# A mixture-of-experts kernel in which the second layer's first tile takes in the last routing of the first layer, and in which two and three tiles may start before all rows are there

## The chip, the cores and the metric

The kernel runs on one core of a Trainium2 chip. A core has five engines with an instruction stream each: PE (TensorE, matrix products; PEld is its weight load), DVE (VectorE), ACT (ScalarE), POOL (GpSimd) and SP (SyncE, which here only issues DMAs). Engines meet by semaphores. The metric is the device time of one execution in microseconds (us), lower is better.

## The reference

Three stages follow each other on 14336 tokens (4 batches of 3584) of 192 features. First a causal convolution of 7 taps, with softmax weights, one set of taps for each of 8 groups of features:

```python
w = exp(weight - max); w = w / (sum(w) + 1e-9)
x[b, s, head h] = sum_k w[h, k] * x_pad[b, s + k, head h]
```

Then a first layer of 8 experts, which only tokens with a positive skip score go through (the others pass unchanged), and a second layer of 8 experts for all tokens:

```python
# layer one, only where x @ w_skip > 0
e = argmax(x @ w_gate);  p = softmax(x @ w_gate)[e]
x = x + p * (relu(x @ w1[e]) @ w2[e])
# layer two, all tokens
e = argmax(x @ w_gate2); p = softmax(x @ w_gate2)[e]
out = p * sigmoid(x @ w_output_gate)[e] * (relu(x @ w1b[e]) @ w2b[e])
```

w1 is 192 x 1024 and w2 is 1024 x 192 for each expert, all float32. Each expert's tokens must be known before its products can be made in tiles, so both layers sort tokens by expert.

## The kernel before, in words

The program has three parts.

**The front** takes the tokens in 16 groups (4 batches of 4) of 7 x 128 tokens. For a group PE does the convolution (`conv`), ACT copies it to the buffer `rows` (`rows_out`, L521), PE transposes it and multiplies by the routers, ACT copies the scores (L557), PE turns them back (`scores_of`), DVE finds the expert, the gate and, with counts from PE (`ranks_of`), the row in a bucket that each token goes to (L703 to L763), and POOL scatters the rows to the buckets in HBM, with 7 indirect DMAs of 128 rows a group (L440). There are 16 buckets, 8 for layer one and 8 for layer two (tokens that skip layer one go straight to the second 8). `rows` has four buffers and `slot_i`, the list of row numbers, has two, so DVE waits at L762 for the scatters of two groups before, and ACT at L524 for those of four groups before. PE and ACT work one group ahead, and so a 17th group is convolved and copied at the end of the front, whose result nothing uses (L1030, L552, L322, L1043). In the last two batches the weights of the first two experts are prepared beside it (`last_batches`). 88 small products that nothing uses keep PE busy before the first convolution (L980).

**Layer one** (m = 0 in the code) then takes its buckets in tiles of 256 rows, in order of the expert. After the front DVE computes a table with each expert's last tile and offset (`tables`, L771 to L794), which every engine reads into registers. With this kernel's inputs layer one has 33 tiles and layer two 60 (3 and 8 in their first buckets). After three batches layer one's first bucket holds 549 rows, and after all four layer two's first holds 841. For tile g SP loads the rows transposed by blocks with 6 DMAs (`load_prep`, L327), DVE transposes the blocks (`x_turn`), ACT and DVE split them in a high and a low part (`x_high`, `x_low`), PE makes the first layer of products (L1095, L1104), ACT the relu (L615), DVE its low part (`h_low`, L821), PE the second layer (L1119, L1126) and DVE the result (`result`). The rows of tile g-1 are routed for layer two beside tile g: PE transposes and scores them after the first half of the first products (`transpose_y`, L1054; `scores`), DVE chooses the expert (`choose`), PE ranks them (`ranks`, L1072), DVE finds the places (`places`, L878), and POOL sends them (L461). On DVE `x_turn` of tile g+1 comes ahead of `choose` of tile g, and on PE `ranks` stands at three quarters of the second products. After the last tile, its rows are routed with nothing beside them (L943 to L947 on DVE, L1134 to L1138 on PE).

**Layer two** (m = 1) needs no routing; its rows go out to their tokens with an indirect DMA each (L466).

SP has one stream for all of its loads. Within a layer its order is, for tile g: `all_there` (first_filled and every scatter landed, L351), the wait for `x_trans` (the buffer is free), `load_prep`, and from an expert's second tile on one of four pieces of the weights of the expert after next (L387), the rest after the expert's last tile (L389). Ahead of a layer it writes filler rows after the end of each bucket (`fill_bucket`, L256), so that a last tile that is not full holds rows that are sent nowhere; SP fills 6 buckets for layer one and 2 for layer two, ACT the others. Tile 0 may be loaded before `all_there`, when its bucket already holds 256 rows three quarters of the way (L343 to L345). After the 33 tiles of layer one, SP, DVE and ACT load, transpose and split one tile more (bucket 0's first, L395), which nothing uses.

## Time and profile before

| | us |
|---|---|
| median of 3 runs (lowest, highest) | 1117.85 (1116.25, 1118.25) |
| the profiled execution, its own time | 1117.96 |
| its span, first to last instruction | 1116.2 |
| PE busy | 1048.8 (94%) |
| DVE busy | 704.9 (63%) |
| ACT busy | 528.4 (47%) |
| POOL busy | 381.1 (34%) |

The front lies from 0 to about 160 us, layer one from 164 to 550, layer two from 555 to the end. Lines named L... are lines of the kernel before. "Busy" of PE counts a product that overlaps the next one, so a full PE shows as 100%.

### The profile page before, as it was taken

The page shows a single profiled execution, that of the slowest core. Times are in us where ns is not written, and L with a number is a line of the kernel's source. Part 1 is how long each engine was busy: PE and PEld are TensorE (multiplying, and loading weights), DVE is VectorE, ACT ScalarE, POOL GpSimd, SP SyncE. Part 2 cuts the span into 40 slices and gives each one's busy share as a digit, 9 for nine tenths or more (in the row PEclk, how much of TensorE's full clock was granted, in tenths as well). Part 3 has the DMA queues.
Part 4 walks back from the last instruction along what each step waited for, and adds up shares of the span by engine and source line. Part 5 has one row for each costly group of instructions (what it writes and reads, how often), then busy time and mean ns, then how long its engine had stood idle before and what let it go on. Part 6 is the DMA issues. An engine that isn't in the chain of part 4 may idle for free.

```text
span 1116.2 us, 32024 instructions
## 1 busy us (share of the span) xinstructions
PE 1048.8 (94%) x8478; PEld 988.4 (89%) x8479; DVE 704.9 (63%) x2258; ACT 528.4 (47%) x1190; POOL 381.1 (34%) x420
## 2 busy tenths in 40 slices
PE   7887747999999999999699999999999999999997
PEld 6666636999999999999599999999999999999997
DVE  1556654887878888888655555565656555565554
ACT  3445532444545454544245454554545455455443
POOL 2677773232323333333222232222323223223212
PEclk9999977999999999999899999999999999999999
DMA  7855334443433344344253343433434343323222
GB/s 209 241 184 156 101 121 117 98 101 71 96 75 93 89 97 98 82 95 110 71 131 81 75 114 65 113 81 79 113 79 111 64 101 93 65 58 73 61 60 49
DMA packets 252866, 110.90 MB, mean 99 GB/s; under 512 B 170515, under 2 KB 247814, under 8 KB 252848
## 3 DMA queue, kind: packets, MB, share of 16 engines
q1 hardware_dynamic: 210344, 62.19, 26.7%
q0 software_dynamic: 14560, 27.96, 7.1%
q10 hardware_dynamic: 27944, 20.57, 6.8%
q14 instruction: 13, 0.11, 0.0%
q8 instruction: 5, 0.08, 0.0%
HBM read 79.48 MB, written 33.08 MB: 101 GB/s over the span
## 4 chain that ended last, share of the span: by engine, by line
PE 83%; issue 7%; POOL 5%; DVE 2%; ACT 1%; DMA 1%; ACTq 1%; POOLq 0%; SPq 0%; DVEq 0%
PE bank L1104 32%; PE bank L1119 26%; PE bank L1126 12%; PE bank L1095 5%; POOL buckets L440 5%; PE bank L1066 2%; PE bank L1065 1%; PE bank L1054 1%; PE bank L1055 1%; PE bank L963 1%; PE bank L982 1%; DMA buckets<-rows,slot_i 0%; PE bank L1026 0%; ACT rows L527 0%; PE bank L1027 0%
## 5 line engine op out<-in xcount | busy, mean ns | idle before, releaser
L1119 PE MATMUL bank<-w,hh 128*128 128x384 f32 x1488 | 444.4, 361 | 0.4 <-DVE hl L821 0.4
L1126 PE MATMUL bank<-w,hl 128*128 128x192 f32 x1488 | 363.9, 255 | 0.0
L821 DVE SCALAR_TENSOR_TENSOR hl<-bank,hh 128x512 fp32r<-128x512 f32 x372 | 252.8, 690 | 126.7 <-ACT hh L615 123.9
L615 ACT ACTIVATE hh<-bank 128x512 fp32r<-128x512 f32 x372 | 221.6, 599 | 161.0 <-PE bank L1104 147.4
L1126 PEld LDWEIGHTS bank<-w,hl 128*128 128x128 f32 x1488 | 282.9, 191 | 0.0
L1119 PEld LDWEIGHTS bank<-w,hh 128*128 128x128 f32 x1488 | 280.4, 188 | 1.5 <-DVE hl L821 0.6
L466 POOL DMA_INDIRECT out<-y_rows,out_i x120 | 117.3, 978 | 413.4 <-DVE out_i L899 382.1
L1104 PE MATMUL bank<-xAh,w1h 128*128 128x256 f32 x744 | 222.5, 299 | 0.0
L1104 PE MATMUL bank<-xAh,w1l 128*128 128x256 f32 x744 | 210.2, 283 | 0.0
L1104 PE MATMUL bank<-xB,w1h 128*128 128x256 f32 x744 | 208.8, 281 | 0.0
L1104 PE MATMUL bank<-xAl,w1h 128*128 128x256 f32 x744 | 208.4, 280 | 0.0
L1104 PEld LDWEIGHTS bank<-xAh,w1h 128*128 128x128 f32 x744 | 142.0, 191 | 12.8 <-issue 0.7
L1104 PEld LDWEIGHTS bank<-xAh,w1l 128*128 128x128 f32 x744 | 142.0, 191 | 0.0
L1104 PEld LDWEIGHTS bank<-xAl,w1h 128*128 128x128 f32 x744 | 141.5, 190 | 0.0
L1104 PEld LDWEIGHTS bank<-xB,w1h 128*128 128x128 f32 x744 | 141.1, 190 | 0.0
L440 POOL DMA_INDIRECT buckets<-rows,slot_i x112 | 110.5, 987 | 57.2 <-issue 33.5
L461 POOL DMA_INDIRECT buckets<-s_rows,slot_i x68 | 66.9, 984 | 175.6 <-DVE slot_i L878 152.3
L567 ACT CAST xAh<-xT 128x256 fp32r<-128x256 f32 x95 | 38.6, 407 | 162.1 <-DVE xT L809 162.1
L897 DVE SCALAR_TENSOR_TENSOR y_rows<-bank,xkeep,y_part 128x192 f32<-128x192 f32 x186 | 68.6, 411 | 33.2 <-ACT y_part L586 33.2
L814 DVE TENSOR_TENSOR xAl<-xT,xAh 128x256 fp32r<-128x256 f32 x95 | 40.5, 426 | 75.0 <-ACT xC L569 75.0
L586 ACT ACTIVATE y_part<-bank,xkeep 128x192 f32<-128x192 f32 x120 | 44.0, 417 | 88.3 <-PE bank L1119 88.3
L1095 PE MATMUL bank<-xB,w1l 64*128 64x256 f32 x372 | 69.7, 308 | 14.2 <-DVE xB L815 14.2
(157 smaller groups left out, 1367.2 us busy)
## 6 DMA issues: line engine op xcount, KB each, us to landing
xblocks<-buckets SPq DMA_DIRECT2D x570, 32.0 KB, 1.8
xkeep<-buckets ACTq DMA_DIRECT2D x93, 196.0 KB, 2.7
xwin<-x SPq DMA_DIRECT2D x17, 672.0 KB
raw<-w_all SPq DMA_DIRECT2D x56, 192.0 KB
raw<-w_all SPq DMA_DIRECT2D x56, 128.0 KB
raw<-w_all SPq DMA_DIRECT2D x112, 64.0 KB
out<-y_rows,out_i POOLq DMA_INDIRECT x120
buckets<-rows,slot_i POOLq DMA_INDIRECT x112
```

Source lines behind the costliest of these rows:

```text
L440: nc.gpsimd.indirect_dma_start(out=buckets, out_offset=bass.IndirectOffsetOnAxis(ap=slot_i[0:W, q % 2, t:t + 1], axis=0), in_=rows[0:W, q, ...
L461: nc.gpsimd.indirect_dma_start(out=buckets, out_offset=bass.IndirectOffsetOnAxis(ap=slot_i[:, 0, h:h + 1], axis=0), in_=s_rows[:, h, :], i ...
L466: nc.gpsimd.indirect_dma_start(out=out, out_offset=bass.IndirectOffsetOnAxis(ap=out_i[:, h:h + 1], axis=0), in_=y_rows[:, h, 0:D], in_offs ...
L586: nc.scalar.mul(y_part[:, h, :], bank[Y[h]][:, 0:D], xkeep[:, h, GATE:GATE + 1]).then_inc(s["y_part"], 1)
L615: nc.scalar.activation(hh[:, 2 * c:2 * c + 2, :].rearrange("p c t -> p (c t)"), bank[c][:], ACT.Relu).then_inc(s["h_high"], 1)
L814: nc.vector.tensor_tensor(xAl[:], xT[:, 0, :], xAh[:].bitcast(F32), ALU.subtract)
L821: nc.vector.scalar_tensor_tensor(hl[:, 2 * c:2 * c + 2, :].rearrange("p c t -> p (c t)"), bank[c][:], 0.0, h, ALU.max, ALU.subtract).then_ ...
L897: nc.vector.scalar_tensor_tensor(y_rows[:, h, 0:D], bank[Y[h]][:, D:2 * D], gated, y_part[:, h, :], ALU.mult, ALU.add)
L1095: nc.tensor.matmul(bank[c + rows_at][:, u * T:(u + 1) * T], w1l[k0, par, 1, at * 128:(at + 1) * 128], (xB, xC)[rows_at][k0, :], start=(u = ...
L1104: last = nc.tensor.matmul(o, w[:, par, half_, f], xs[:], start=False, stop=(i == 3), skip_group_check=True)
L1119: return nc.tensor.matmul(bank[Y[h]][:, 0:2 * D], hh[:, j, t], w2[:, par, j, :, :].rearrange("p a d -> p (a d)"), start=(j == 0), stop=(j ...
L1126: last = nc.tensor.matmul(bank[Y[h]][:, 0:D], hl[:, j, t], w2[:, par, j, 0, :], start=False, stop=False)
```

## The change

1. *Transition.* Layer two's tile 0 is taken out of its loop and put at the end of layer one's code, on PE, ACT and DVE, with the routing of layer one's last tile in it where a tile of layer one has that of the tile before. What SP loads after the last tile of layer one is now layer two's tile 0. The table of layer two is computed behind this routing, still before `result` of the tile. SP then loads tiles 1 and 2 of layer two before it waits for the table, fills all 8 buckets itself (ACT none), and waits for `all_there` only from tile 3 on.
2. *Early tiles.* `EARLY = (2, 3)`: five stretches of 256 rows (two in layer one's first bucket, three in layer two's) are filled with filler rows at the start by POOL, which waits for them to land before it scatters. Tiles 0 and 1 of layer one may be loaded when 3 of 4 batches are scattered. The next free row of these two buckets is raised to the end of the stretch where it would be less.
3. *Slots.* `slot_i` has four buffers and the wait at L762 is gone; layer one's places have a tile of their own (`slot2_i`).
4. *Scatters.* The 112 scatters of the front have no `bounds_check`.
5. *Front.* The 17th group is gone on PE, ACT and SP; layer one's first `send`, of rows that go nowhere, is gone. PE does 112 useless products before the first convolution and 24 after it.

```diff
-            sp.wait_ge(conv_ready, (B - 1) * GPB + 1)
-            load_windows(0, 0)
@@ SP, ahead of each layer
                 if m == 0:
-                    sp.wait_ge(counted, B - 1)
+                    sp.wait_ge(raised, 1)
+                    sp.wait_ge(prefilled, 16 * sum(EARLY))
                     for q in range(GPB):
                         sp.wait_ge(scattered[q], 16 * WPG * (B - 1 + (1 if q else 0)))
+                    load_prep(0, 0)
                 else:
                     n0 = last_tile(sp, 0)
                     sp.wait_ge(mix_sems[0]["x_trans"], n0 + 1)
                     settle(sp)
-                there = sp.value_load(count_i[0:1, m:m + 1], min_val=0, max_val=CAP)
-                with sp.If(there > T - 1):
-                    load_prep(0, m * E * CAP)
+                    load_prep(1, E * CAP)
+                    sp.wait_ge(s["x_trans"], 2)
+                    load_prep(2, E * CAP)
                 sp.wait_ge(tables_ready, m + 1)
                 fill_bucket(sp, m, 0, first_filled)
                 for e in range(1, SP_FILLS[m]):      # SP_FILLS is now (6, E)
                     fill_bucket(sp, m, e, filled)
@@ SP, in a layer's loop
-                            with sp.If(g > 0):
+                            with sp.If(g > EARLY[m] - 1):
                                 all_there()
+                            with sp.If(g > (0, 2)[m]):
                                 sp.wait_ge(s["x_trans"], g)
                                 load_prep(g, off)
                             with sp.If(g > first):
                                 pieces.one()
@@ POOL
+            pool.wait_ge(consts_pool, 12)
+            for m in range(2):
+                for t in range(EARLY[m]):
+                    pool.dma_start(bass.AP(buckets.tensor, (m * E * CAP + t * T) * ROW, [[SUB * ROW, 128], [1, SUB * ROW]]),
+                                   filler[:].rearrange("p s c -> p (s c)")).then_inc(prefilled, 16)
+            pool.wait_ge(prefilled, 16 * sum(EARLY))
@@
-                            out=buckets, out_offset=bass.IndirectOffsetOnAxis(ap=slot_i[0:W, q % 2, t:t + 1], axis=0),
-                            in_=rows[0:W, q, t, :], in_offset=None,
-                            bounds_check=NB * CAP - 1, oob_is_err=False).then_inc(scattered[q], 16)
+                            out=buckets, out_offset=bass.IndirectOffsetOnAxis(ap=slot_i[0:W, q, t:t + 1], axis=0),
+                            in_=rows[0:W, q, t, :], in_offset=None).then_inc(scattered[q], 16)
@@ DVE, front
-                    dve.wait_ge(scattered[(q + 2) % GPB], b * (16 * WPG) + 16 * WPG * (1 if q < 3 else 2))
-                    nc.vector.tensor_copy(slot_i[0:W, q % 2, :], slot[0:W]).then_inc(slots_ready, 1)
+                    nc.vector.tensor_copy(slot_i[0:W, q, :], slot[0:W]).then_inc(slots_ready, 1)
@@ DVE, after layer one's loop
-                    for part in (flags, choose, gate, places):
-                        part(step, n)
+                    h_low(0, 0, s1)
+                    flags(step, n)
+                    for c in range(1, PAIRS):
+                        h_low(0, c, s1)
+                    x_turn(1, s1, 1)
+                    choose(step, n)
+                    x_low(1, s1)
+                    gate(step, n)
+                    places(step, n)
+                    tables(1)
+                    result(0, s1, 1)
@@ PE, front and after layer one's loop
-            with pe.Fori(0, 11):
+            with pe.Fori(0, 14):
...
+            warm(24)
...
-                    transpose_y(n)
+                    weights_ready(E)
+                    pe.wait_ge(s["xT_ready"], n + 2)
+                    settle(pe)
+                    first_layer(0, s1, lambda: transpose_y(n))
                     scores(n)
-                    ranks(n)
+                    pe.wait_ge(s1["yrows_ready"], 1)
+                    second_layer(0, s1, 0, lambda: ranks(n))
```

Three places show how instructions move. The first is SP's stream between the two layers, before the change (`xblocks` are the loads of a tile, `table` the read of the table into a register, `filler` the fill of a bucket; layer two's loop follows the second fill):

```order
L330 DMA xblocks<-buckets 32x8x32 [waits m0_x_trans]
L330 DMA xblocks<-buckets 32x8x32 x5
L343 TENSOR_LOAD count_i [waits m0_x_trans]
L343 ISA x2
L344 COMPARE_AND_BRANCH
L330 DMA xblocks<-buckets 32x8x32 x6
L258 TENSOR_LOAD table [waits tables_ready]
L259 DMA buckets<-filler 128x392
```

and after it:

```order
L329 DMA xblocks<-buckets 32x8x32 [waits m0_x_trans]
L329 DMA xblocks<-buckets 32x8x32 x5
L329 DMA xblocks<-buckets 32x8x32 [waits m0_x_trans]
L329 DMA xblocks<-buckets 32x8x32 x5
L329 DMA xblocks<-buckets 32x8x32 [waits m1_x_trans]
L329 DMA xblocks<-buckets 32x8x32 x5
L259 TENSOR_LOAD table [waits tables_ready]
L260 DMA buckets<-filler 128x392
```

The loads of tiles 1 and 2 now stand ahead of the wait for the table, and the read and fill at the end stand there eight times where they stood twice.

The second is DVE at the same place, after the change (before, the routing from `flag` to `slot_i` stood alone, then the table, and the loop followed):

```order
L853 SCALAR_TENSOR_TENSOR hl<-bank,hh 128x512 [waits m1_h_high] x3
L840 STREAM_TRANSPOSE xT<-xblocks 128x256 [waits m1_prep_in]
L841 STREAM_TRANSPOSE xT<-xblocks 64x256
L869 TENSOR_REDUCE top<-bank 128x2 [waits m0_scores]
L846 TENSOR_TENSOR xAl<-xT,xAh 128x256 [waits m1_x_high]
L909 TENSOR_TENSOR slot_i<-slot,flag 128x2 [waits m0_step]
L821 CAST table<-tile_f 1x8 [waits table_step]
L928 SCALAR_TENSOR_TENSOR y_rows<-bank,xkeep,y_part 128x192 [waits m1_sent,m1_y_part,m1_y_ready,m1_keep_in]
```

The table now lies behind tile 0's low parts and the places, and ahead of its result (the small tile `slot2_i` stands under the name `slot_i`).

The third is POOL's stream between its constants and the first scatters, after the change (before, the first row was followed directly by the scatters):

```order
L433 DMA spare<-weight_rev 8x7 x3
L437 DMA buckets<-filler 128x392 [waits consts_pool]
L437 DMA buckets<-filler 128x392 x4
L441 UNCONDITIONAL_BRANCH [waits prefilled]
L446 DMA buckets<-rows,slot_i 245760x196 [waits slots_ready]
L446 DMA buckets<-rows,slot_i 245760x196 x6
```

Five fills and one wait for their landing are new ahead of the first scatter.

## Rows read from the trace of the kernel before

**Rows 1.** Windows: start:end, length, busy per engine, granted PE clock, DMA share, GB/s.
```profile
15.27:18.80 3.53, 3.52 (x15) 3.39 (x16) 0.25 (x2) 1.06 (x2) 0.00 (x0) 0.52 1.00 300
...
555.20:561.50 6.30, 6.25 (x32) 6.02 (x33) 0.00 (x0) 0.00 (x0) 0.00 (x0) 0.50 0.63 206
...
200.00:540.00 340.00, 340.00 (x2666) 324.18 (x2665) 277.62 (x1034) 163.40 (x364) 109.31 (x121) 1.00 0.39 90
```

**Rows 2.** Line L440: durations in ns (min/median/max), first and last start.
```profile
L440 POOLq MOVE  x112: 29/29/38, 30.3 to 162.7; - x112
L440 POOL DMA_INDIRECT buckets<-rows,slot_i x112: 978/980/1223, 31.2 to 174.5; - x112
```

**Rows 3.** Line L434, POOL's plain DMAs, the same columns.
```profile
L434 POOL DMA_DIRECT2D spare<-weight_rev x3: 518/518/518, 6.3 to 7.3; - x3
```

**Rows 4.** Timeline of the front's start: start, length, instruction, idle before.
```profile
23.34 0.32 PE L1026 MATMUL bank<-ident,rows 128*128 128x128 f32 x1 [0.67 <-ACT rows L527]
...
31.15 0.32 PE L1026 MATMUL bank<-ident,rows 128*128 128x128 f32 x1 [0.67 <-ACT rows L527]
```

**Rows 5.** Timeline of PE from the front's end to layer one's fourth tile.
```profile
151.82 0.57 PE L1006 MATMUL bank<-ident,scoreT 128*128 128x128 f32 x2 [2.08 <-ACT scoreT L557]
...
164.43 0.58 PE L1095 MATMUL bank<-xB,w1l 64*128 64x256 f32 x1 [8.61 <-DVE xB L815]
...
184.04 0.20 PE L1072 MATMUL bank<-hot_pad,before 128*128 128x24 bf16 x1 [7.77 <-DVE score L851]
...
198.91 0.38 PE L1095 MATMUL bank<-xB,w1l 64*128 64x256 f32 x1
...
210.01 0.38 PE L1095 MATMUL bank<-xB,w1l 64*128 64x256 f32 x1
```

**Rows 6.** Timeline of DVE in the same stretch.
```profile
159.15 0.18 DVE L763 CAST slot_i<-slot 128x7 int32<-128x7 f32 x1 [1.12 <-DMA buckets<-rows,slot_i]
...
161.55 0.45 DVE L808 STREAM_TRANSPOSE xT<-xblocks 128x256 f32<-128x256 f32 x1 [0.16 <-DVE table L793]
...
181.92 0.45 DVE L808 STREAM_TRANSPOSE xT<-xblocks 128x256 f32<-128x256 f32 x1 [9.01 <-DMA xblocks<-buckets]
```

**Rows 7.** Timeline of SP's queue in the same stretch.
```profile
162.14 6.68 SPq L259 DMA_DIRECT2D buckets<-filler  x6
177.54 2.92 SPq L330 DMA_DIRECT2D xblocks<-buckets  x6
...
185.16 2.87 SPq L330 DMA_DIRECT2D xblocks<-buckets  x6
188.91 1.86 SPq L233 DMA_DIRECT2D raw<-w_all  x3
...
192.60 1.83 SPq L233 DMA_DIRECT2D raw<-w_all  x3
...
200.91 9.06 SPq L330 DMA_DIRECT2D xblocks<-buckets  x12
```

**Rows 8.** Timeline of PE at the transition between the layers.
```profile
542.75 0.36 PE L1119 MATMUL bank<-w,hh 128*128 128x384 f32 x1
...
555.25 0.58 PE L1095 MATMUL bank<-xB,w1l 64*128 64x256 f32 x1 [5.60 <-DVE xB L815]
...
567.89 0.38 PE L1095 MATMUL bank<-xB,w1l 64*128 64x256 f32 x1
```

**Rows 9.** Timeline of DVE at the same place.
```profile
542.97 0.16 DVE L878 TENSOR_TENSOR slot_i<-slot,flag 128x2 int32<-128x2 f32 x1
...
551.03 0.15 DVE L779 SCALAR_TENSOR_TENSOR tile_i<-next_row,bucket_row 1x8 int32<-1x8 f32 x1
...
552.38 0.45 DVE L808 STREAM_TRANSPOSE xT<-xblocks 128x256 f32<-128x256 f32 x1
```

**Rows 10.** The chain that ended last, two tiles of layer two: start, length, line.
```profile
577.82 3.94 PE bank L1104 x32
587.00 3.94 PE bank L1104 x32
```

More of the change, by code:

```diff
@@ L56, in program @@
     BIG = float(NB * CAP)
-    MAXT = N // T + E
+    MAXT = N // T + E + max(EARLY)
     XB = D // 32
@@ L359, in all_there @@
                         settle(sp)
-                with sp.If(there < T):
-                    all_there()
-                    load_prep(0, m * E * CAP)
                 tiles = Tiles(sp, m)
@@ L485, in _ @@
                             if m == 0:
-                                send(g, pieces.one)
+                                with pool.If(g > 0):
+                                    send(g, pieces.one)
                             else:
@@ L507, in _ @@
             prime(act, mix_sems[0]["yT_copied"])
+            prime(act, mix_sems[1]["x_high"], 3)
             act.wait_ge(kern_step, 2)
@@ L551, in _ @@
                             exp_of(n - 1)
-                    rows_out(n + 1, (q + 1) % GPB)
+                    if q < GPB - 1:
+                        rows_out(n + 1, q + 1)
+                    else:
+                        with act.If(b < B - 1):
+                            rows_out(n + 1, 0)
                     act.wait_ge(scores_ready, n + 1)
@@ L579, in exp, with h_high, y_half @@
                                          ACT.Exp).then_inc(s["e"], 1)
-                def y_half(g):
+                def h_high(g, c, s=s):
+                    act.wait_ge(s["h_ready"], g * PAIRS + (c + 1))
+                    nc.scalar.activation(hh[:, 2 * c:2 * c + 2, :].rearrange("p c t -> p (c t)"),
+                                         bank[c][:], ACT.Relu).then_inc(s["h_high"], 1)
+                def y_half(g, s=s):
                     act.wait_ge(s["keep_in"], g * 16 + 16)
@@ L592, in _ @@
                     fill_bucket(act, m, e, filled)
-                tiles = Tiles(act, m)
+                tiles = Tiles(act, m, m)
                 with act.Fori(0, E // 2) as half:
@@ L634, in _ @@
                     n = last_tile(act, m)
-                    yT_copy(n)
+                    s1 = mix_sems[1]
+                    act.wait_ge(s["y_ready"], n + 1)
+                    settle(act)
+                    for c in range(PAIRS):
+                        h_high(0, c, s1)
+                        if c == 1:
+                            act.wait_ge(s["yrows_ready"], n + 1)
+                            settle(act)
+                            act.dma_start(xkeep[:], tile_rows(0, E * CAP)).then_inc(s1["keep_in"], 16)
+                            yT_copy(n)
+                    x_high(1, s1)
                     exp(n)
+                    y_half(0, s1)
         @block.vector
@@ L979, in _, with warm @@
             pe.wait_ge(ones_ready, 1)
-            with pe.Fori(0, 11):
-                for _ in range(8):
+            def warm(n):
+                for _ in range(n):
                     nc.tensor.matmul(bank[7][:, 0:128], ones[:], ones[:], start=True, stop=True)
+            with pe.Fori(0, 14):
+                warm(8)
             pe.wait_ge(win_zero, 3)
@@ L1008, in scores_of, with next_group @@
                 last.then_inc(scores_ready, 1)
+            def next_group(q, b, part):
+                if q < GPB - 1:
+                    part(b * GPB + (q + 1), q + 1)
+                else:
+                    with pe.If(b < B - 1):
+                        part(b * GPB + (q + 1), 0)
             def last_group(q, b, part):
@@ new lines, in second_layer, with high_terms @@
+                def second_layer(par, s, g, between):
+                    for j in range(FC):
+                        if j % 2 == 0:
+                            pe.wait_ge(s["h_low"], g * PAIRS + (j // 2 + 1))
+                        for h in range(SUB):
+                            t = slice(h * 128, (h + 1) * 128)
+                            def high_terms():
+                                return nc.tensor.matmul(
+                                    bank[Y[h]][:, 0:2 * D], hh[:, j, t],
+                                    w2[:, par, j, :, :].rearrange("p a d -> p (a d)"),
+                                    start=(j == 0), stop=(j == FC - 1))
+                            if j == 0:
+                                high_terms()
+                            last = nc.tensor.matmul(bank[Y[h]][:, 0:D], hl[:, j, t], w2[:, par, j, 0, :],
+                                                    start=False, stop=False)
+                            if j > 0:
+                                last = high_terms()
+                        if j == 5:
+                            between()
+                    last.then_inc(s["y_ready"], 1)
```

149 lines of the change are left out of this document (71 added, 78 removed).

## The prediction

> **What bounds the kernel now.** I read the windows first, for PE and its clock. From 200 to 540 us PE is busy for all 340 us at a granted clock of 1.00 (2.4 GHz) [rows 1]: inside the two layers nothing but PE's own work sets the time, 11.10 us a tile in layer one (198.91 to 210.01) [rows 5] and 9.18 us in layer two [rows 10]. So the change can only act where PE stands idle, at the front and between the layers.
>
> The front I read on POOL and then on the others. Its 112 scatters run from 31.2 to 174.5 us, 1.291 us apart, each 0.98 us long [rows 2]: POOL never rests. The other engines could go faster: at the start, before the buffers are full, a group takes PE 7.8 us (23.34 to 31.15) [rows 4], and POOL 9.04 us. So POOL sets the front's pace, through the `rows` buffers. After it PE has tile 0 from 164.43, stands from 176.3 to 184.04, and begins tile 2 at 198.91 [rows 5]: the load of tile 1 waits for the last scatter and goes out at 177.54 [rows 7].
>
> Between the layers PE ends layer one at 543.1, begins layer two's tile 0 at 555.25 and its tile 1 at 567.89 [rows 8].
>
> **Transition, as PE sees it.** Layer two's tile 0 now follows at 543.2, with the last routing in it. It is a tile of layer one's kind, 11.1 us, and ends at 554.3. Its rows are there: SP's load after the last tile stood in the same place before, and its bucket holds 841 rows from the front. Before, the same point was 567.89. That would be 13.6 us.
>
> What is late next is the table. DVE's nine table instructions took 1.3 us (551.03 to 552.38) [rows 9] and stand behind `places`. In the trace `slot_i` of a tile is written at PE's end of that tile (543.13 and 543.11) [rows 8, 9]; without a weight piece in this tile I put it 0.4 us earlier, at 553.9. So the table is written at T = 555.2. PE needs it before tile 1. No row has PE's time from table to product; SP's from table to its first fill is 0.75 us (161.39 to 162.14) [rows 6, 7], and DVE's, which reads no register, 0.16 [rows 6]. I take 1.0, with 0.2 and 2 as bounds. Tile 1 starts at T + 1.0 = 556.2, and PE has been idle for 1.9 us. Whether it then starts at the lower clock makes no difference, since tile 3 waits for another reason (below).
>
> The Trainium skill (DMA: Bandwidth & Descriptors, section on latency and other measured facts) gives a `tensor_load` a floor of about 600 ns. No run here shows it for PE; by it the 0.2 us end would fall away, and the sum would stay.
>
> **Transition, as SP sees it.** This decides most of what is kept. SP loads tiles 1 and 2 a tile ahead each. But for tile 3 it goes through this, all behind the table:
> - 8 fills where there were 2 (ACT's 6 are now SP's). Six took 6.68 us from 0.75 us behind the table [rows 6, 7], so eight take 8.9: T + 9.7.
> - the entry to the loop with two reads of the table. At an expert's end, from the start of its last-but-one weight piece to the next tile load, SP took 8.3 us (192.60 to 200.91) [rows 7], of which two pieces with their gap are 6.1; 2.2 remain: T + 11.9.
> - tiles 1 and 2 load nothing there, but each issues a piece of weights, 3.69 us apart (188.91 to 192.60) [rows 7]: T + 19.2.
> - the six loads of tile 3; from the first issue to DVE's transpose 4.4 us (177.54 to 181.92) [rows 6, 7]: T + 23.6. From there to PE's start 2.9 us (161.55 to 164.43) [rows 5, 6]: T + 26.5.
>
> PE wants to start tile 3 at T + 1.0 + 2 x 9.18 = T + 19.4. It stands for 7.1 us, whatever T is. And it then starts cold: before, after 5.6 us of idleness the granted clock was 0.50 (1.2 GHz) for 6.3 us [rows 1, 8], which costs half of that, 3.1 us. Tile 3 ends at T + 26.5 + 9.2 + 3.1 = T + 38.8 = 594.0. Before, tile 3 ended at 567.89 + 3 x 9.18 = 595.4. **The transition gives 1.4 us**, not 13.6. Bounds: 11.7 if SP keeps up (13.6 less 1.9 for the table), and -1 if the fills take 1.3 us each and the pieces 4.
>
> **The end of the front, with POOL as it is.** Without the 17th group ACT no longer waits for a `rows` buffer ahead of the last scores, and the 2.08 us that PE stood for them go [rows 5]. Without the `slot_i` wait 1.12 us go [rows 6]. The table of layer one, ready at 161.39 [rows 6], comes 3.2 us earlier: t = 158.2. (The other waits for `slot_i` before it are hidden by POOL.) What follows, from t:
> - PE starts tile 0 at t + 3.0 and reaches `ranks` at t + 14.9 (176.3 less 161.39) [rows 5].
> - SP ends its six fills at t + 7.4 and enters the loop by t + 9.6; tile 1's load goes out there, since it need not wait for the last batch. DVE transposes at t + 14.0, and `ranks` can run 2.1 us later (181.92 to 184.04) [rows 5, 6], at t + 16.1. PE stands 1.2 us.
> - The last quarter of the second products takes 1.3 us (my estimate: 4 pairs of the 16 in about 5 us). Tile 1 starts at t + 17.4 and tile 2 at t + 28.5 = 186.7. Before, 198.91: 12.2 us.
>
> What is late next: tile 2's load goes out when the last scatter has landed, 177.54 as before [rows 7], and tile 3's 15.75 us behind it (185.16 to 200.91: a piece, the two remaining pieces of the first expert, the loop's end) [rows 7], at 193.3, so PE gets tile 3 at 193.3 + 4.4 + 2.9 = 200.6 instead of 186.7 + 11.1 = 197.8. That takes 2.8 us back, some less when POOL is faster: I take 2.0. Before, this was hidden, because PE was later.
>
> **The scatters.** No row has an indirect DMA without the check. From below 0; from above 0.46 us each, the difference to a plain DMA of 8 rows, 518 ns [rows 3]. Nearest is the register write before each scatter, 29 ns [rows 2], which I take to be the limit for the check: I take 0.03 in all. Through the buffers it is the end of group 11, 84 scatters, that sets the table: 84 x 0.03 = 2.5 us. More than 0.17 a scatter is no use, since the others need 7.8 us a group [rows 4]: 14.4 us at most.
>
> The Trainium skill (DMA: Bandwidth & Descriptors, SWDGE vs HWDGE vs iDMA) says that for POOL's DMAs a program computes one pair of descriptors per operation. By it the 0.98 us are the 128 rows' descriptors and the check next to nothing, and the sum would be 2.5 us less; the difference between 518 and 980 ns agrees in sign.
>
> **The first scatter.** For: from 15.27 to 18.80 PE ran at a mean granted clock of 0.52 with the DMA share at 1.00 [rows 1]; 24 products there keep it warm, and half of 3.5 us, 1.7, is to be had. Against: 5 x 200 KB of fills share the DMA engines with the windows and weights; at the 300 GB/s of that row they take 3.4 us. POOL issues them by about 12 us (five at 0.5 to 1.0 us behind the three at 6.3) [rows 2, 3], and they must have landed by 31. I take +0.5, from +1.7 to -4. Layer one's first `send` and the smaller `slot` waits in the layers lie beside PE's work: nothing.
>
> **Sum.** 12.2 - 2.0 + 2.5 + 0.5 + 1.4 = 14.6 us, against the profiled execution's 1117.96: 1103.4. It is 0.1 from the median of 1117.85, so I say 1103.4.
>
> **Rivals.**
> 1. *SP keeps up at the transition.* The reads and fills run closer than at the front, or the pieces do. For it: only one stretch has six fills by SP. Against: a piece at the first expert was 3.7 us apart with nothing to wait for. The transition gives up to 11.7 instead of 1.4: about 1093 to 1096.
> 2. *The check was dear.* At 0.1 us a scatter 8.4 instead of 2.5 us, at 0.17 14.4: 1097.5 to 1091.5. For it: half of a scatter's time is not explained by a plain DMA. Against: 128 rows instead of 8 explain it.
> 3. *The early tiles come to little.* SP's fills and table reads before tile 1's load take 4 us longer or the landing of the loads is slow beside POOL's scatters, so that PE stands cold before tile 1 too: 4 us and 3 of clock: about 1110.
> 4. *The fills hold up the first scatter, and the kernel is slower.* DMA shares are at 1.00 from 15 us on [rows 1], and POOL now waits there. Every us that the fills land after 31.2 is a us of the whole. From 46 us on, 15 us late, the change is a loss; at 48 the time would be 1120. For it: a full queue. Against: 1 MB at a full share needs 3.4 us and is issued early.
>
> **Numbers.** Forecast 0.50, its own range 1099 to 1107; rival 1 0.19; rival 2 0.16; rival 3 0.11; rival 4 0.04. The range 1089 to 1110 leaves out both rivals 1 and 2 together, the worse half of rival 3, and rival 4. Less than 0.2%, 2.2 us, can't be told from no change; faster 0.95, same 0.01, slower 0.04.
>
> **What would show it.** POOL's first scatter at 30 to 31.5 and the last starting at 170 to 172. DVE's table of layer one at about 155. PE idle 1 to 2 us ahead of `ranks` in tile 0, and 1 to 3 us ahead of tile 3. At the transition no gap but about 2 us ahead of tile 1, and then 6 to 8 us ahead of tile 3 with eight fills and two pieces in SP's queue before the six loads, and a granted clock of 0.50 behind it. If PE has no gap before tile 3, or the scatters lie under 1.2 us apart, the time is well under 1100; if the first scatter is after 35, over 1107.

## The result, and the profile after

| | before | after |
|---|---|---|
| median us (lowest, highest), beside each other on one chip | 1117.98 (1116.25, 1118.25) | 1109.90 (1109.67, 1110.46) |
| the profiled execution, its own time | 1117.96 | 1109.67 |
| its span | 1116.2 | 1107.9 |
| mean granted TensorE clock | 0.976 | 0.981 |

The ratio of after to before is 0.9931 (95%: 0.9915 to 0.9947). The kernel is 8.1 us faster, where 14.6 was forecast: 1109.9, at the slow end of the range (1089 to 1110) and outside the forecast's own 1099 to 1107. PE's busy time did not move (1048.8 and 1048.7 us); all of the difference is idle time and cold clock. Ratios, here and below, leave out slow executions, those over 1.5% above the fastest of their kernel (of pieces late, for one, 1138.3 us at a granted clock of 0.839, where its others had 0.983 to 0.985). In this part L numbers are those of the kernel that is shown.

**The front, from the first scatter.** One line's durations in ns (min/median/max), first and last start, as in [rows 2]:

```profile
L446 POOL DMA_INDIRECT buckets<-rows,slot_i x112: 956/961/1080, 31.3 to 172.6; - x112
```

The first scatter starts where it did, and the last 1.9 us earlier. From first to last there were 143.3 us, now 141.3: 0.018 us less for each of 111 steps (0.03 forecast). Timeline of POOL and of PE at the start (start, length, instruction, idle before):

```profile
7.87 2.73 POOL L437 DMA_DIRECT2D buckets<-filler  x5
31.32 1.03 POOL L446 DMA_INDIRECT buckets<-rows,slot_i  x1 [20.71 <-DVE slot_i L790]
```
```profile
17.86 1.41 PE L1004 MATMUL bank<-xwin,toep 128*128 128x168 f32 x8 [1.14 <-DMA xhalo<-x]
```

POOL ends issuing the five fills 20 us before DVE's first list of rows is there, so they hold up no scatter. PE, now at a granted clock of 1.00 from 15.27 to 18.80 us (0.52 before), then waits 1.14 us for its input, and the first scatter gains nothing. Before, the same product began at 17.01 without a wait, so its input now comes at least 0.85 us later. Whether the five fills among the transfers do that, no run separates.

**From the table of layer one to its fourth tile.** t is the time of the table, 0.16 us ahead of DVE's first `xT`. Timelines of DVE, SP and PE, to be read beside [rows 5 to 7]:

```profile
156.87 0.45 DVE L840 STREAM_TRANSPOSE xT<-xblocks 128x256 f32<-128x256 f32 x1
...
172.96 0.45 DVE L840 STREAM_TRANSPOSE xT<-xblocks 128x256 f32<-128x256 f32 x1 [4.75 <-DMA xblocks<-buckets]
...
197.27 0.45 DVE L840 STREAM_TRANSPOSE xT<-xblocks 128x256 f32<-128x256 f32 x1 [0.44 <-DMA xblocks<-buckets]
```
```profile
157.73 6.64 SPq L260 DMA_DIRECT2D buckets<-filler  x6
168.22 2.95 SPq L329 DMA_DIRECT2D xblocks<-buckets  x6
...
176.09 2.87 SPq L329 DMA_DIRECT2D xblocks<-buckets  x6
...
191.99 9.10 SPq L329 DMA_DIRECT2D xblocks<-buckets  x12
```
```profile
175.08 0.20 PE L1124 MATMUL bank<-hot_pad,before 128*128 128x24 bf16 x1 [3.49 <-DVE score L883]
177.60 0.58 PE L1140 MATMUL bank<-xB,w1l 64*128 64x256 f32 x1
190.34 0.38 PE L1140 MATMUL bank<-xB,w1l 64*128 64x256 f32 x1
...
201.44 0.38 PE L1140 MATMUL bank<-xB,w1l 64*128 64x256 f32 x1
```

t is 156.7, 4.7 us earlier than before (6.2 forecast). SP's fills end at t + 7.7 (7.4 forecast), but its entry to the loop takes 3.85 us where 2.2 were forecast, and the load of tile 1 goes out only at t + 11.5 (9.6 forecast). DVE therefore has tile 1 at t + 16.3, and since this transpose stands ahead of `choose` on DVE, PE waits 3.49 us at `ranks` (1.2 forecast) and goes on at half the clock; tile 1 takes 12.7 instead of 11.1 us. Tile 3, the first before which PE neither waits nor runs cold, starts at 201.44 against 210.01: the front's end gives 8.57 us, where 13.2 were forecast (12.2 - 2.0 + 2.5 + 0.5).

**Between the layers.** T is layer two's table, ready at about 546.5. Timelines of SP, PE and DVE, to be read beside [rows 8 to 10]:

```profile
547.67 8.29 SPq L260 DMA_DIRECT2D buckets<-filler  x8
559.93 1.89 SPq L234 DMA_DIRECT2D raw<-w_all  x3
562.23 0.42 SPq L236 DMA_DIRECT2D raw<-w_all  x1
564.19 2.50 SPq L234 DMA_DIRECT2D raw<-w_all  x3
567.07 0.40 SPq L236 DMA_DIRECT2D raw<-w_all  x1
568.52 2.87 SPq L329 DMA_DIRECT2D xblocks<-buckets  x6
```
```profile
548.15 0.38 PE L1140 MATMUL bank<-xB,w1l 64*128 64x256 f32 x1 [2.50 <-issue]
557.33 0.38 PE L1140 MATMUL bank<-xB,w1l 64*128 64x256 f32 x1
575.85 0.58 PE L1140 MATMUL bank<-xB,w1l 64*128 64x256 f32 x1 [9.27 <-DVE xB L847]
```
```profile
572.98 0.45 DVE L840 STREAM_TRANSPOSE xT<-xblocks 128x256 f32<-128x256 f32 x1 [9.61 <-DMA xblocks<-buckets]
```

The gap of 5.6 us ahead of layer two is down to 2.50, and PE then stands 9.27 us ahead of tile 3. SP's queue has the forecast's parts in the forecast's order: eight fills, two pieces of weights, six loads. The fills end where they should (T + 9.5, 9.7 forecast), but from there to the first piece it is 4.0 us where 2.2 were forecast, and the two pieces are 4.3 us apart instead of 3.7. Windows (start:end, length, busy per engine, granted clock, DMA share, GB/s) show what follows the two stalls, and the stretch after the second:

```profile
177.60:182.00 4.40, 4.40 (x26) 4.17 (x26) 1.98 (x6) 0.60 (x1) 0.51 (x1) 0.58 0.40 77
575.80:582.00 6.20, 6.15 (x36) 5.92 (x37) 2.82 (x6) 2.21 (x5) 2.99 (x3) 0.61 0.49 107
582.00:590.00 8.00, 8.00 (x64) 7.68 (x63) 4.27 (x10) 4.34 (x10) 0.68 (x1) 1.00 0.41 90
```

Tile 3 of layer two takes 11.33 us (tile 4 starts at 587.18) instead of 9.18. The same tile began at 595.45 before, so 8.27 us are gained here in all, 8.57 of them in the front: the transition costs 0.3 us instead of giving 1.4.

### The profile page after: what moved, and what is told of

Read it like the earlier page. It is cut to its first block, busy times and chain, and to the rows that moved or that the text cites. A ratio compares the mean times of both kernels' runs of the same rounds, so it can differ in the third digit from the quotient of the medians.

```text
span 1107.9 us, 31973 instructions
## 1 busy us (share of the span) xinstructions
PE 1048.7 (95%) x8494; PEld 988.0 (89%) x8495; DVE 703.5 (64%) x2252; ACT 526.0 (47%) x1183; POOL 381.4 (34%) x422
## 4 chain that ended last, share of the span: by engine, by line
PE 82%; SPq 2%; issue 1%; DVE 0%; DMA 0%; ACT 0%; POOLq 0%; ACTq 0%; DVEq 0%; POOL 0%
PE bank L1149 33%; PE bank L1163 26%; PE bank L1170 12%; PE bank L1140 6%; PE bank L1118 2%; PE bank L1117 1%; PE bank L1106 1%; PE bank L1107 1%; SPq L329 0%; SPq L234 0%; DMA xblocks<-buckets 0%; SPq L259 0%; SPq L260 0%; PE bank L1126 0%; SPq L236 0%
```

## The experiments

Theory A: SP's one queue makes the tiles late, at both places. Rival B: what ends the waits is the landing of rows or another engine. Rival C: what is gained is given back at a later tile.

On three occasions every kernel, the one before too, took about 1200 us (before: 1205.1, 1204.6 and 1211.0 median). Most of it lies in the front: in the traces of those runs t comes 58 to 75 us later than in the kernel after, layer one takes 16 to 32 us more, and in the control layer two 8 us more. The profile calls many of the short waits of PE in that front "issue". Eleven runs have this slow front: the control, the first three of pieces late and of tile 1 ahead, fills late, both of pieces and fills late, and the first of all three. They price nothing, but their traces have the same chain in them and are read for it. One of the three chips gave the usual times later.

**The control: the kernel after, once more.** No edit.

> The kernel after, unchanged, beside the others on the same chip, to compare with. Both theories: 1109 to 1112, as before.

1210.6 us beside 1204.6 for before, ratio 1.0126 (0.9980 to 1.0272). Whether the change gains anything where the front is this slow can't be told. The stall is there: table at 640.3, tile 3's load at 664.12.

```profile
671.46 0.58 PE L1140 MATMUL bank<-xB,w1l 64*128 64x256 f32 x1 [8.28 <-DVE xB L847]
```

**Pieces late.** Layer two's weight pieces start with tile 3.

```diff
-                            with sp.If(g > first):
-                                pieces.one()
+                            if m == 0:
+                                with sp.If(g > first):
+                                    pieces.one()
+                            else:
+                                with sp.If(g > 2):
+                                    with sp.If(g > first):
+                                        pieces.one()
```

> Layer two's weight pieces start only with tile 3 (the two behind the skipped loads of tiles 1 and 2 come later). Theory A (SP's queue is what is late for tile 3): in the kernel after, the two pieces stand at 559.93 and 564.19, 4.3 us apart, and the load of tile 3 at 568.52. Without them it goes out at about T + 13.5 = 560, 8.5 us earlier; the 9.3 us that PE stood before tile 3 come down to about 0.7, PE stays at a granted clock of 1.00 there and the 2.2 us of cold clock go too: 10 to 11 us in all, about 1099, unless the pieces are then late for the third expert. Rival B (what ends the wait is not the queue but the data: last scatters or sends landing, all_there): tile 3's load stays at about T + 22 and the time at 1109 to 1110. Rival C (given back: the fill-less weights arrive late and PE stands at a later tile): the stall before tile 3 goes, the time stays above 1105.

> The kernel of e1_pieces_late again, on a chip on which the kernel before takes its usual time: layer two's weight pieces only from tile 3 on. Theory A (SP's queue makes tile 3 late): tile 3's load goes out 8.5 us earlier, PE's stall of 9.3 us and 2.2 us of cold clock go: 1099 to 1101. Rival B (landing of the last rows ends the wait): 1109 to 1110. Rival C (later tiles give it back): over 1105.

> Layer two's weight pieces only from tile 3 on, to price it. In the slow-front trace of the same kernel PE had no stall before tile 3 and a clock of 0.97 over the stretch, where the kernel after stood 9.3 us and ran at 0.6 behind it. Theory A (SP's queue): 9 to 11.5 us less than after, 1099 to 1101. Rival C (given back later): 1105 or more. Rival B (the stall only belongs to the landing of data): 1109 to 1110.

> Layer two's weight pieces only from tile 3 on, to price it where the front takes its usual 150 us. Theory A (SP's queue): 9 to 11.5 us less than after, 1099 to 1101. Rival C (given back at later tiles): 1105 or more. Rival B (landing of data): 1109 to 1110.

The first three had the slow front: 1207.5, 1205.3 and 1198.6 us, ratios 1.0040 (0.9995 to 1.0085) and 1.0033 (0.9976 to 1.0089), the third without an interval. In their traces the longest wait of PE for tile data at this place is 2.0, 2.5 and 2.4 us, where the control has 8.3. The fourth gave **1100.74 us, ratio 0.9831 (0.9809 to 0.9854)**, 9.2 us less than the median of after, which was measured on another occasion (by the two ratios, each to the kernel before beside it, 11 us less). SP, PE, and a window of the same tile:

```profile
547.46 8.29 SPq L260 DMA_DIRECT2D buckets<-filler  x8
560.85 2.92 SPq L329 DMA_DIRECT2D xblocks<-buckets  x6
564.60 1.88 SPq L234 DMA_DIRECT2D raw<-w_all  x3
```
```profile
547.91 0.38 PE L1145 MATMUL bank<-xB,w1l 64*128 64x256 f32 x1 [2.47 <-issue]
558.65 0.38 PE L1145 MATMUL bank<-xB,w1l 64*128 64x256 f32 x1
568.70 0.38 PE L1145 MATMUL bank<-xB,w1l 64*128 64x256 f32 x1 [0.79 <-DVE xB L852]
```
```profile
568.70:575.00 6.30, 6.30 (x53) 6.17 (x54) 4.63 (x9) 3.35 (x7) 2.99 (x3) 1.00 0.54 123
```

The load goes out 7.7 us earlier, PE stands 0.79 us, the clock stays at 1.00, and no later tile gives it back: after tile 3 PE has no wait in the rest of layer two. Theory A holds here, B and C fall. Tile 4 starts at 577.89 against 587.18, 9.3 us earlier (0.5 of them from layer one), which is the difference of the two profiled times (1109.67 less 1100.37). Tile 1 took 10.74 us instead of 9.18, at a lower clock for a part, and that costs nothing, since PE still waits for tile 3.

**Fills late.** Seven of the eight fills stand behind tile 3's load.

```diff
-                for e in range(1, SP_FILLS[m]):
-                    fill_bucket(sp, m, e, filled)
+                if m == 0:
+                    for e in range(1, SP_FILLS[m]):
+                        fill_bucket(sp, m, e, filled)
...
                                 load_prep(g, off)
+                            if m == 1 and par == 0:
+                                with sp.If(g > 2):
+                                    with sp.If(g < 4):
+                                        for e2 in range(1, SP_FILLS[m]):
+                                            fill_bucket(sp, m, e2, filled)
```

> Layer two's fills of buckets 1 to 7 stand behind tile 3's load instead of ahead of the loop. Theory A: eight fills took from T + 1.2 to T + 9.5, 8.3 us; seven of them go from ahead of tile 3's load, about 7.5 us with their table reads, so PE's stall of 9.3 us comes down to about 2 us, and the cold clock behind it mostly goes: 7.5 to 9.5 us, 1100 to 1102. Rival B (all_there or the landing of data ends the wait): same time, 1109 to 1110. Rival C (the table reads and fills only move): tile 4's load is then late by the same 7.5 us, and half or more is given back: 1105 to 1109.

1217.7 us with the slow front, ratio 1.0119 (1.0040 to 1.0198). Its PE rows at tiles 3 and 4, and SP's between them:

```profile
660.53 0.38 PE L1146 MATMUL bank<-xB,w1l 64*128 64x256 f32 x1 [1.97 <-DVE xB L853]
676.66 0.58 PE L1146 MATMUL bank<-xB,w1l 64*128 64x256 f32 x1 [6.89 <-DVE xB L853]
```
```profile
652.99 3.20 SPq L329 DMA_DIRECT2D xblocks<-buckets  x6
657.14 6.98 SPq L260 DMA_DIRECT2D buckets<-filler  x7
665.64 1.86 SPq L234 DMA_DIRECT2D raw<-w_all  x3
667.89 0.42 SPq L236 DMA_DIRECT2D raw<-w_all  x1
669.38 2.87 SPq L329 DMA_DIRECT2D xblocks<-buckets  x6
```

The wait only moves: 2.0 us before tile 3, and 6.9 before tile 4, whose load now stands behind the fills. SP has to be free of the fills' time by tile 4 too. This is rival C, for this edit; no run of it with the usual front says what it costs.

**Pieces and fills late.** Both edits.

> Both edits: no pieces and one fill instead of eight ahead of tile 3's load. Theory A: 16 us less in SP's queue than the kernel after; only 9.3 are wanted, so it is no faster than the one with late pieces alone by more than its remaining stall (0.7 us): PE has no stall at all before tile 3, and 1098 to 1100. If the fills then make tile 4's load late, 1100 to 1103. Rival B: 1109 to 1110.

> The kernel of e3_both_late again: late pieces and seven fills behind tile 3's load. Theory A: no stall before tile 3; 1098 to 1100, or 1100 to 1103 if the fills make tile 4's load late. Rival B: 1109 to 1110.

1207.7 and 1202.1 us with the slow front, ratios 1.0056 (1.0019 to 1.0094) and 0.9995 (0.9942 to 1.0049). No wait is left before tile 3 and one of 2.9 to 3.0 us is there ahead of tile 4: again the fills.

**Tile 1 ahead.** Layer one's tile 1 is loaded ahead of the table and the six fills.

```diff
                     load_prep(0, 0)
+                    sp.wait_ge(s["x_trans"], 1)
+                    load_prep(1, 0)
...
-                            with sp.If(g > (0, 2)[m]):
+                            with sp.If(g > (1, 2)[m]):
```

> Layer one's tile 1 is loaded directly behind tile 0 (behind the wait for its buffer), ahead of the table and SP's six fills. Theory A (SP's queue makes tile 1 late in the front's end): the load went out at t + 11.5, DVE's transpose at t + 16.3, and PE stood 3.49 us ahead of ranks and then ran from 177.6 to 182 at a granted clock of 0.58. With tile 1 there, PE stands at most 0.3 us and stays warm: 3.3 + 1.6, about 5 us of which tile 3, whose load waits behind the last scatter and the pieces, gives 1 to 2 back: 1105 to 1107. Rival B (DVE, or the buffer, or DMA contention is what was late): PE's wait ahead of ranks stays over 2 us and the time at 1109 to 1110. Rival C (tile 2 or 3 takes all of it back): PE's wait goes, and shows again ahead of tile 2 or 3.

> The kernel of e4_tile1_ahead again: layer one's tile 1 is loaded ahead of the table and SP's fills. Theory A: PE's 3.5 us ahead of ranks and the cold clock behind it go, 1 to 2 us come back at tile 3: 1105 to 1107. Rival B (buffer, DVE or contention): 1109 to 1110. Rival C: the wait shows again ahead of tile 2 or 3, and the time stays within 1 us of 1110.

> Layer one's tile 1 loaded ahead of the table and the fills, to price it. In the slow-front trace PE's wait ahead of ranks in tile 0 was gone, but tile 2 had one of 1.8 us ahead of its ranks-point, since its load and tile 3's stand where they stood (behind the pieces and the last scatters). Theory A: 3.5 us and about 1.8 of cold clock gained; rival C: since tile 3's load goes out when it did before, most comes back there. From the slow-front traces tile 2 to tile 3 now takes the time up: the load of tile 3 was at 265 in both. I now lean to C: 1 to 3 us less than after, 1107 to 1109; theory A alone 1105.

> Layer one's tile 1 loaded ahead of the table and the fills, to price it. Rival C (the load of tile 3 goes out when it did, so most comes back there): 1 to 3 us less than after, 1107 to 1109. Theory A (all of it is kept): 5 us, 1105. Rival B (other cause): 1109.5 to 1110.5.

With the slow front 1211.6, 1209.2 and 1201.3 us (ratios 1.0033, 0.9988 to 1.0077, and 1.0068, 1.0020 to 1.0116; the third without). With the usual one **1110.37 us, ratio 0.9928 (0.9901 to 0.9956)**: no difference from after, where 1107 to 1109 was expected. PE, SP, DVE and the last scatter of that run:

```profile
172.89 0.38 PE L1142 MATMUL bank<-xB,w1l 64*128 64x256 f32 x1
...
184.31 0.38 PE L1142 MATMUL bank<-xB,w1l 64*128 64x256 f32 x1
...
199.47 0.20 PE L1126 MATMUL bank<-hot_pad,before 128*128 128x24 bf16 x1 [5.14 <-DVE score L885]
...
202.00 0.58 PE L1142 MATMUL bank<-xB,w1l 64*128 64x256 f32 x1
```
```profile
161.50 6.11 SPq L260 DMA_DIRECT2D buckets<-filler  x6
172.12 1.98 SPq L234 DMA_DIRECT2D raw<-w_all  x3
...
176.31 2.88 SPq L329 DMA_DIRECT2D xblocks<-buckets  x6
...
192.92 8.26 SPq L329 DMA_DIRECT2D xblocks<-buckets  x12
```
```profile
197.35 0.44 DVE L842 STREAM_TRANSPOSE xT<-xblocks 128x256 f32<-128x256 f32 x1 [6.39 <-DMA xblocks<-buckets]
```
```profile
172.38 0.96 POOL L448 DMA_INDIRECT buckets<-rows,slot_i  x1 [0.30 <-issue]
```

Theory A's mechanism is there: the wait of 3.49 us is gone, and tile 1 starts 4.7 us earlier and tile 2 6.0 us earlier than in the kernel after. And rival C takes all of it: tile 3's load goes out when it did (192.92 against 191.99), PE stands 5.14 us at tile 2's `ranks` instead, goes on cold, and starts tile 3 at 202.00 (201.44). The chain that sets the front's end here is SP's queue from the table on: the rest of tile 1's load, the fills (now 3.8 us later), tile 1's piece of weights, tile 2's load, the pieces, tile 3's load 16.6 us later, DVE's transpose 4.4 us after that, and 4.65 us to PE's start. It isn't the last scatter: tile 2's load follows its start by 3.9 us (3.5 in the kernel after), where 3.0 were enough before and 2.9 in "tile 1 waits" below, and the trace shows no wait of SP for it.

The equal time hides two differences. Tile 3 runs cold for a part, so that tile 4 of layer one starts at 214.65 against 212.54 and layer two's table is 2.6 us late. Between the layers 1.6 us of that come back, in code that the edit leaves alone: SP's queue brings tile 3 of layer two 1.2 us sooner behind the table, and the cold part of that tile is 0.5 us shorter.

**All three.**

> Late pieces and late fills in layer two and tile 1 ahead in layer one, together. If the two places are independent, the sum of the single gains: 9 to 11.5 at the transition and 1 to 3 at the front's end, 1096 to 1100. If the transition's part is not gained (rival C there), 1103 or more.

> All three together. By the kernel with late pieces alone (0.983 of before, about 1100), and 1 to 3 us for tile 1: 1097 to 1100. If the late fills make tile 4 of layer two late, or tile 3 of layer one takes tile 1's gain back, 1100 to 1102.

1199.9 us with the slow front (before: 1211.0). With the usual one 1106.91 us, ratio 0.9906 (0.9876 to 0.9937): slower than pieces late alone (1097 to 1102 was expected). Against after it is 3.0 us less by the medians, but the intervals of the ratios overlap, so a gain isn't shown. Layer two's table is ready 1.4 us later than in pieces late alone, which leaves tile 3 0.5 us late, and the fills hold up tile 4:

```profile
581.36 0.39 PE L1153 MATMUL bank<-xB,w1l 64*128 64x256 f32 x1 [2.86 <-DVE xB L860]
```

Tile 4 then takes 10.70 us instead of 9.18, at a lower clock for a part. The three, 0.5, 2.9 and 1.5 us, make up the 5.0 us between the two profiled times. The miss is mine: the trace of fills late already had this wait.

**The terms of the front, one at a time.** Four kernels beside each other on one chip, on which before took 1119.2 us.

```diff
# check back: each of the front's scatters
+                            bounds_check=NB * CAP - 1, oob_is_err=False
# tile 1 waits: layer one's tile 1 waits for all scatters
-                            with sp.If(g > EARLY[m] - 1):
+                            with sp.If(g > (0, 2)[m]):
                                 all_there()
# group 17 back (the same on PE, and SP's windows for it)
-                        with act.If(b < B - 1):
-                            rows_out(n + 1, 0)
+                        rows_out(n + 1, 0)
# slot wait back, the four buffers kept
+                    dve.wait_ge(scattered[(q + 2) % GPB], b * (16 * WPG) + 16 * WPG * (1 if q < 3 else 2))
                     nc.vector.tensor_copy(slot_i[0:W, q, :], slot[0:W])
```

> The 112 scatters of the front have their bounds check back, all else as after. From the two traces the pitch of the scatters went from 1.291 to 1.273 us, 0.018 us each; over the 84 that set the end of group 11 that is 1.5 us: 1111.4. Prediction's own figure 0.03 each: 2.5 us, 1112.4. Rival (the difference of the pitches has another cause than the check): under 0.5 us, and the register write in front of each scatter (29 ns) comes back without costing time.

> Layer one's tile 1 waits for all scatters again, as before the change, though its stretch is filled early. The last scatter started at 172.6 and lands about 2 us later, so tile 1's load goes from 168.2 to about 175, DVE's transpose to about 180, PE's wait ahead of ranks from 3.5 to 10 us: +6.8 us, less what tile 3 then need not wait: 1114 to 1117. Rival (the early tile 1 came to little since tile 2 and 3 are bound by the last scatter anyway): under 2 us, 1110 to 1112.

> The 17th group, which nothing uses, is convolved and copied again at the end of the front. The prediction's term: PE stood 2.08 us ahead of the last scores because ACT waited for a rows buffer. Main: the table of layer one comes 2 us later and with it all of layer one: 1112. If the last scatter bounds tile 2 and 3 anyway, about 1 us: 1111. Rival (ACT's copy also delays further work, cold clock): over 3 us.

> DVE waits for the scatters of two groups before ahead of each slot_i again, with four buffers all the same. Before, DVE waited 1.12 us for it at the last group. Main: this wait ends before or with the one that ACT has on the rows buffers, except in the last group, where it costs 1.1 us: 1111. Rival (the wait hides behind POOL, which is the bound through the whole front): 0, 1110. Rival 2 (in every group the wait holds DVE and with it the next group's slots): 3 us or more.

| | median | ratio to before (95%) | t | tile 3 of layer one starts |
|---|---|---|---|---|
| after (measured apart) | 1109.90 | 0.9931 (0.9915 to 0.9947) | 156.7 | 201.4 |
| check back | 1112.24 | 0.9938 (0.9921 to 0.9956) | 159.9 | 204.4 |
| tile 1 waits | 1115.60 | 0.9968 (0.9957 to 0.9980) | 156.6 | 208.7 |
| group 17 back | 1111.19 | 0.9930 (0.9913 to 0.9946) | 158.0 | 202.0 |
| slot wait back | 1111.99 | 0.9936 (0.9919 to 0.9952) | 159.8 | 204.1 |

By the ratios only "tile 1 waits" differs from after: 0.0037, about 4 us; by the medians 5.7, by the traces at tile 3 7.3 (PE stands 10.31 us at tile 0's `ranks` instead of 3.49). Of the four, the early tile is the largest part of the gain. For the others the intervals reach over after's, and the traces say more. One line of check back, and its columns as above:

```profile
L446 POOL DMA_INDIRECT buckets<-rows,slot_i x112: 978/980/1465, 31.0 to 175.6; - x112
```

With the check a scatter takes 980 ns instead of 961, and the 111 steps take 144.6 instead of 141.3 us, 0.030 each: the prediction's figure, and tile 3 is 3.0 us later. DVE's row of slot wait back:

```profile
157.46 0.17 DVE L791 CAST slot_i<-slot 128x7 int32<-128x7 f32 x1 [2.20 <-DMA buckets<-rows,slot_i]
```

The wait costs 2.2 us here (1.1 was expected) and tile 3 is 2.7 us later. Group 17 costs 1.2 us at t and 0.6 at tile 3. The delays of t, 3.2, 1.2 and 3.1 us, sum to more than the 4.7 by which the change moved t, so together they cost less than one by one. Each rests on one trace.

## Why the prediction was wrong

- *What bounds, and which side.* Right: PE's work did not change, the gain is idle time and clock, and it lies in the front's end and not in the transition.
- *The transition.* Right in mechanism, place and order, and off in size. The fills were right (T + 9.5 for 9.7). The entry to the loop was taken from the passage between two experts, 2.2 us, and took 4.0, so the first piece went out at T + 13.4 (11.9). The two pieces were 4.26 us apart (3.69), the load went out at T + 22.0 (19.2), and the stall was 9.3 (7.1). The cold clock cost 2.15 instead of 3.1, and PE started tile 1 at T + 1.6 instead of 1.0. In all -0.3 instead of +1.4. That the queue is the cause is shown by pieces late: without two pieces in it the stall goes and 9.2 us are gained.
- *The failed step: "SP ends its six fills at t + 7.4 and enters the loop by t + 9.6 ... PE stands 1.2 us. ... Tile 1 starts at t + 17.4".* This is where the sum for the front's end went wrong. The entry to the loop took 3.85 us instead of 2.2, as it took 4.0 at the transition, and the load of tile 1 went out 1.9 us late. PE stood 3.49 us instead of 1.2, and the cold clock behind the stall, for which the sum had nothing, cost 2.8 (1.2 in the last quarter, 1.6 in tile 1). With t itself 1.5 us late, and less the 2.0 that the sum had set aside for tile 3 and that was not needed (PE has no wait there), tile 3 came 4.6 us later than forecast: 201.4 for 196.8. Why the entry takes 1.6 to 1.8 us longer than the passage between two experts is open.
- *The second step that failed: "What is late next ... PE gets tile 3 at 193.3 + 4.4 + 2.9 = 200.6 ... I take 2.0".* This chain was named, but with the faster scatters and the earlier first one in the sum it too was to end at 196.8. In the kernel after it would have let PE have tile 3 at 201.1 (191.99 + 4.43 + 4.65, the last two from tile 1 ahead), 0.4 us before PE was there, so that mending tile 1 alone could give no more than about that. Its 4.3 us are three terms. Tile 2's load went out at 176.1 instead of 173.7, 1.9 of it since the last scatter came only 1.9 us earlier (3.8 in the sum), and 0.5 since SP's queue, and no longer the scatter, was what came last. Tile 3's load was 15.9 us behind it instead of 15.75. And from DVE's transpose to PE's start it is 4.65 us instead of 2.9, because the transpose stands ahead of tile 2's `choose`, so that `ranks` and the last quarter of tile 2 come behind it (1.1 us of this is the cold clock of that quarter). Tile 1 ahead showed this chain alone: 202.0.
- *Tile 1 of layer one.* This is rival 3 (given 0.11), with its time, about 1110, and it did set the time of the kernel after: the chain that ended last runs through this tile's load and `ranks`. But rival 3 puts the miss on this tile alone, and taking the stall away changed nothing (1110.4), since tile 3's chain ends within 0.4 us of it.
- *The scatters.* 0.018 us from the traces of before and after, 0.030 from check back against after, for 0.03 forecast: the size was about right, rival 2 (0.1 or more) is excluded. From what the Trainium skill (DMA: Bandwidth & Descriptors, SWDGE vs HWDGE vs iDMA) says, that for POOL's DMAs a program computes a pair of descriptors for each operation, the prediction had worked out a check that costs next to nothing and a sum 2.5 us less. The check is small but not nothing: 19 ns of duration in 980, and the 29 ns register write before each is gone.
- *Group 17 and `slot_i`.* Forecast 3.2 us at t, and 6.2 with the scatters and the first one; measured 4.7. By the traces of before and after 0.6 of the missing 1.5 is the first scatter and 1.0 the pitch (84 x 0.018 instead of 2.5). Put back alone, each part costs 1.2 to 3.2 us at t.
- *Rival 1 and rival 4* did not come: SP did not keep up, and the fills were issued by 10.6 us and landed 3.3 us behind their issue (median), long before 31.3.
- *The range.* It reached 1110 by a hair. The transition's lower bound, -1, came from longer fills and pieces and held; for the front's end only rival 3 stood for a later SP, and the range left out its worse half. Where one queue serves at two places, its lateness adds up at both.

**The better version** is pieces late alone: 1100.74 us, ratio 0.9831 to before. Left open: whether tile 3 of layer one can be loaded ahead of the first expert's remaining pieces, which by the traces hold the front's end once tile 1 is in time; and how SP's fills could be taken from ahead of tile 4.

## What to carry to other kernels

When a stall goes, write down for each of the next three tiles when its load can leave the queue and when the engine wants it; the gain ends at the first that is later, and repairing an earlier one may give nothing (tile 1 ahead: 0 us). A queue that prefetches weights and tiles by turns needs a rule for a catch-up phase: two pieces issued where no tile was due cost 9 us here, and moved by two tiles cost nothing. Price the entry to a loop where the loop is entered (3.9 and 4.0 us here), not where it goes on to its next round (2.3 us). Behind a load, count what the program order puts behind its first consumer too, not only the way to the next tile.

## What was not expected of the hardware

- *The clock after a short gap.* PE stood 2.47 to 2.52 us ahead of layer two's tile 1 in every run with the usual front. In after and in slot wait back the granted clock stayed at 1.00 (2.4 GHz) and the tile took 9.18 us; in check back, tile 1 waits, pieces late and all three it took 10.7 (10.74 us at 0.84 in pieces late); in group 17 back and in tile 1 ahead it began at half the clock and took 11.9 and 12.0. Windows of after, and of group 17 back:

```profile
548.10:555.00 6.90, 6.85 (x57) 6.72 (x58) 3.44 (x6) 2.51 (x5) 2.31 (x3) 1.00 0.69 233
```
```profile
549.40:556.00 6.60, 6.58 (x35) 6.36 (x36) 1.38 (x2) 1.27 (x3) 2.28 (x3) 0.54 0.63 216
```

The slower tile cost nothing, since tile 3 waited for SP: PE's stall there was 5.08 instead of 9.27 us, 2.7 of the difference from the tile and 1.5 from SP's queue, which was that much quicker behind the table.

```profile
575.66 0.58 PE L1141 MATMUL bank<-xB,w1l 64*128 64x256 f32 x1 [5.08 <-DVE xB L848]
```

The same gap gives either level, so a forecast across such a gap is open by 2 to 3 us.
- *The slow front.* In the control PE's weight loads at L1090 waited 35.1 us for "issue" from 30 to 200 us, against 3.7 us from 30 to 150 in the kernel after. Its table was 70 us later, and layer one took 24 us more and layer two 8. The cause is not known. A comparison needs the kernel before on the same chip at the same time.
